# Thirty-two unused bytes per partition in front of the identity matrix, in an attention kernel with two dense layers

## The chip, the cores and the metric

The kernel runs on one core of one Trainium2 chip. The metric is the device time of one execution in microseconds (us); lower is better.

## What is computed

The reference is windowed attention followed by two dense layers, all in 32-bit floating point:

```python
scores = q @ k.T / sqrt(64)             # q, k, v: (4, 8, 768, 64): batch, heads, positions, width
scores += bias                          # a slope for each head times the distance
scores = where(is_global | is_local, scores, -1e9)   # the first 8 keys, or the last 96
a = softmax(scores)
x = (a @ v)                             # regrouped to 3072 tokens x 512
h = x @ moe_w_in;   g = h * cos(h);     y = g @ moe_w_out       # 512 -> 2048 -> 512
h = y @ moe2_w_in;  g = relu(h) ** 2;   out = g @ moe2_w_out    # 512 -> 2048 -> 512
```

## The kernel before

Nothing is scheduled by a library: every engine has its own program, written by hand (`sync`, `gpsimd`, `tensor`, `scalar`, `vector`), and the programs meet at semaphores. The tokens are cut into 6 tiles of 512 tokens (`TILES`), and the 2048 hidden columns into 16 pieces of 128 (`FC`). One step, numbered F, is one piece of one tile: 96 steps for the first layer, 96 for the second. Two steps are one `pair`.

A step has two parts on TensorE. `up(F)` (L519 to L521) makes 128 hidden columns for 512 tokens. `down(F)` multiplies them by 128 rows of the second weight matrix (L538 to L540 in the first layer, L543 to L545 in the second). Each part issues 12 matmuls of 128 rows by 128 columns by 512: 4 blocks, and 3 products each, because every operand is split into a rounded part ("hi") and the rest ("lo"), and hi*hi, hi*lo and lo*hi are added. These operands have the type float32r. A matmul takes a *stationary* operand of 128 columns, which a weight load puts into the array, and a *moving* operand of 512 columns, which streams through it. In a row of the profile, `psum<-x_parts,w_in_hi` names the moving operand first.

- `up`: moving is `x_parts` (the tokens), stationary are `w_in_hi` and `w_in_lo`.
- `down`, first layer: moving are `g_hi` and `g_lo`, stationary are `w_out_hi` and `w_out_lo`.
- `down`, second layer: moving are `w_out_hi` and `w_out_lo`, stationary are `g_hi` and `g_lo`.

The attention runs in groups G (48 of them, two heads and two blocks of 128 queries each). The first 11 run ahead of the dense layers. The others are laid between the `up` and `down` of the first 37 pairs. Their TensorE work is plain float32: transposes against `ident` (L555, L592, L595), scores (L574, out of the array `kq`) and the product with the values (L610). VectorE makes the argument of the cosine (`angle`, L955 to L961: four instructions a step), the product (`gate`, L967 or L971) and the low part (`low_g`, L975). ScalarE copies the hidden columns out of PSUM, makes the cosine and rounds. GpSimd splits the weights (L425 to L436) and normalises the probabilities (L449). In the second layer `angle` falls away.

The arrays lie in each partition of the on-chip memory in the order in which `sb(...)` names them. In the built program every array starts at a multiple of 32 bytes. `w_in_hi` starts at byte 16,512, which is 129 times 128, and `w_in_lo` at 49,280, which is 385 times 128. Seven small arrays follow (`n_words` to `half_pi`), each of which takes 32 bytes, 224 in all. So `ident` starts at byte 82,272, which is 96 bytes past a multiple of 128. Everything after it that is used here has a size that is a multiple of 128, and so starts 96 past one as well: `raw`, `x_parts0`, `x_parts1`, `w_stage`, `w_out_raw`, `w_out_hi`, `w_out_lo`, `hs`, `turns`, `act_a`, `g_hi`, `g_lo`, `y_stage`, `bias`, `probs`, `probsT`, `kq`, `vals`, `x_raw`. A slice of 512 columns is 2,048 bytes in each partition, and a stationary operand of 128 columns 512 bytes. Within the arrays of the dense layers all slices start at multiples of 512 bytes from the array's start. Within `kq` and `probs` they don't: a row of `kq` is 2,880 bytes (22.5 times 128), a slot of `probs` 928 bytes (7.25 times 128).

Of the kernel before, what the change touches and what calls it, by code (L numbers as in the profile page):

```python
# [11 lines left out]
P = 128  # L12
# [10 lines left out]
def build(nc, q, k, v, n_global, n_local, w1_in, w1_out, w2_in, w2_out, out):  # L23
# [41 lines left out]
    with ExitStack() as ctx:  # L65
        def sb(name, shape, dt=F32, where=ctx):
            return where.enter_context(nc.sbuf_tensor(name, shape, dt))
# [10 lines left out]
        fits = sb("fits", [P, 3])  # L78
        general_flag = sb("general_flag", [P, 1], I32)
        half_pi = sb("half_pi", [P, 1])  # L80
        ident = sb("ident", [P, P])
        raw = sb("raw", [P, 3, 2, 2, 2 * D])

# [1047 lines left out]
```

## Time and profile before

| what | value |
|---|---|
| time, median of 3 runs | 1290.38 us (1289.87 to 1290.68) |
| time of the profiled execution | 1287.4 us |
| its span, first to last instruction | 1285.6 us |
| outside the span | 1.8 us |
| mean granted TensorE clock | 0.996 of full speed |
| TensorE matmul (PE) busy | 1244.2 us, 97% of the span |
| VectorE (DVE) busy | 712.4 us, 55% |
| GpSimd (POOL) busy | 622.6 us, 48% |
| ScalarE (ACT) busy | 562.8 us, 44% |

The busy time of a matmul is counted from its start to its modelled end. Neighbours overlap, so how fast TensorE really goes is read from the distance between two starts, not from the duration of one.

### The profile page before, as it was taken

The page shows a single profiled execution, that of the slowest core. Times are in us where ns is not written, and L with a number is a line of the kernel's source. Part 1 is how long each engine was busy: PE and PEld are TensorE (multiplying, and loading weights), DVE is VectorE, ACT ScalarE, POOL GpSimd, SP SyncE. Part 2 cuts the span into 40 slices and gives each one's busy share as a digit, 9 for nine tenths or more (in the row PEclk, how much of TensorE's full clock was granted, in tenths as well). Part 3 has the DMA queues.
Part 4 walks back from the last instruction along what each step waited for, and adds up shares of the span by engine and source line. Part 5 has one row for each costly group of instructions (what it writes and reads, how often), then busy time and mean ns, then how long its engine had stood idle before and what let it go on. Part 6 is the DMA issues. An engine that isn't in the chain of part 4 may idle for free.

```text
span 1285.6 us, 18074 instructions
## 1 busy us (share of the span) xinstructions
PE 1244.2 (97%) x6240; PEld 991.5 (77%) x6240; DVE 712.4 (55%) x1434; ACT 562.8 (44%) x1164; POOL 622.6 (48%) x687
## 2 busy tenths in 40 slices
PE   5689999999999999999998899999999999999998
PEld 4567777777777777777776778888888888888887
DVE  6568777777767777676789962223222323222222
ACT  4655666666666666666432322222222222222221
POOL 4767455544555544555477753333333333333332
PEclk9999999999999999999999999999999999999999
DMA  4633223323222322231142332131131131321211
GB/s 122 168 87 91 74 65 101 78 64 92 80 69 77 98 73 65 69 101 49 42 143 79 97 101 67 44 114 49 49 115 47 44 115 50 93 71 44 80 49 58
DMA packets 131748, 102.01 MB, mean 79 GB/s; under 512 B 62912, under 2 KB 97856, under 8 KB 131648
## 3 DMA queue, kind: packets, MB, share of 16 engines
q1 hardware_dynamic: 131648, 100.77, 27.7%
q8 instruction: 52, 0.85, 0.3%
q14 instruction: 48, 0.39, 0.1%
HBM read 88.15 MB, written 12.58 MB: 78 GB/s over the span
## 4 chain that ended last, share of the span: by engine, by line
PE 89%; DVE 7%; ACT 2%; POOL 1%; issue 1%; DMA 0%; SPq 0%; DVEq 0%; ACTq 0%; POOLq 0%
PE psum L519 13%; PE psum L521 13%; PE psum L520 13%; PE psum L545 7%; PE psum L543 7%; PE psum L544 7%; PE psum L538 7%; PE psum L540 6%; PE psum L539 6%; PE psum L574 3%; PE psum L610 3%; PE psum L595 2%; PE psum L555 2%; DVE act_a L959 1%; DVE act_a L967 1%
## 5 line engine op out<-in xcount | busy, mean ns | idle before, releaser
L434 POOL TENSOR_SCALAR w_out_hi<-w_out_raw 128x512 fp32r<-128x512 f32 x192 | 141.3, 736 | 605.8 <-PE psum L545 320.3
L519 PE MATMUL psum<-x_parts,w_in_hi 128*128 128x512 f32 x768 | 310.5, 404 | 0.0
L521 PE MATMUL psum<-x_parts,w_in_lo 128*128 128x512 f32 x768 | 304.0, 396 | 0.0
L520 PE MATMUL psum<-x_parts,w_in_hi 128*128 128x512 f32 x768 | 303.2, 395 | 0.0
L436 POOL TENSOR_TENSOR w_out_lo<-w_out_raw,w_out_hi 128x512 fp32r<-128x512 f32 x192 | 263.0, 1370 | 16.0
L975 DVE TENSOR_TENSOR g_lo<-act_a,g_hi 128x512 fp32r<-128x512 f32 x192 | 149.2, 780 | 184.1 <-ACT g_hi L771 180.9
L761 ACT ACTIVATE hs<-psum 128x512 f32<-128x512 f32 x96 | 57.3, 597 | 364.4 <-PE psum L521 364.4
L519 PEld LDWEIGHTS psum<-x_parts,w_in_hi 128*128 128x128 f32 x768 | 144.4, 188 | 37.0 <-issue 6.5
L521 PEld LDWEIGHTS psum<-x_parts,w_in_lo 128*128 128x128 f32 x768 | 144.2, 188 | 34.3
L520 PEld LDWEIGHTS psum<-x_parts,w_in_hi 128*128 128x128 f32 x768 | 144.6, 188 | 31.7
L538 PE MATMUL psum<-g_hi,w_out_hi 128*128 128x512 f32 x384 | 158.7, 413 | 10.0 <-DVE g_lo L975 10.0
L540 PE MATMUL psum<-g_hi,w_out_lo 128*128 128x512 f32 x384 | 151.4, 394 | 0.0
L539 PE MATMUL psum<-g_lo,w_out_hi 128*128 128x512 f32 x384 | 150.8, 393 | 0.0
L545 PE MATMUL psum<-w_out_hi,g_lo 128*128 128x512 f32 x384 | 150.1, 391 | 0.0
L543 PE MATMUL psum<-w_out_hi,g_hi 128*128 128x512 f32 x384 | 149.7, 390 | 0.0
L544 PE MATMUL psum<-w_out_lo,g_hi 128*128 128x512 f32 x384 | 149.4, 389 | 0.0
L449 POOL TENSOR_SCALAR probs<-probs,row_inv 128x232 f32<-128x232 f32 (+1 forms) x192 | 134.3, 717 | 16.5 <-DVE row_inv L928 16.5
L771 ACT CAST g_hi<-act_a 128x512 fp32r<-128x512 f32 x192 | 118.4, 617 | 48.4 <-DVE act_a L971 29.0
L971 DVE TENSOR_TENSOR act_a<-hs 128x512 f32<-128x512 f32 x96 | 65.6, 702 | 88.9 <-ACT hs L761 88.9
L967 DVE TENSOR_TENSOR act_a<-hs,act_a 128x512 f32<-128x512 f32 x96 | 77.0, 837 | 60.0 <-ACT act_a L765 60.0
L759 ACT COPY hs<-psum 128x512 f32<-128x512 f32 x96 | 55.9, 582 | 117.6 <-PE psum L521 117.6
L538 PEld LDWEIGHTS psum<-g_hi,w_out_hi 128*128 128x128 f32 x384 | 72.7, 189 | 35.8 <-issue 22.3
(74 smaller groups left out, 1641.6 us busy)
## 6 DMA issues: line engine op xcount, KB each, us to landing
w_out_raw<-in_moe_w_out_dram SPq DMA_DIRECT2D x192, 256.0 KB, 2.7
vals<-in_v_dram SPq DMA_DIRECT2D x80, 112.0 KB
w_stage<-in_moe_w_in_dram SPq DMA_DIRECT2D x32, 256.0 KB, 3.1
raw<-in_k_dram SPq DMA_DIRECT2D x96, 64.0 KB, 2.4
raw<-in_q_dram SPq DMA_DIRECT2D x96, 64.0 KB, 2.2
y_dram<-y_stage SPq DMA_DIRECT2D x24, 256.0 KB, 3.6
x_raw<-y_dram SPq DMA_DIRECT2D x6, 1024.0 KB, 5.3
out_dram<-y_stage SPq DMA_DIRECT2D x24, 256.0 KB, 3.4
```

What stands on the lines that cost most here:

```text
L434: pool.tensor_scalar(hi, row, 1.0, 1.0, ALU.mult, ALU.mult).then_inc(w_out_hi_ready, 1)
L436: pool.tensor_tensor(lo, row, hi.bitcast(F32), ALU.subtract).then_inc(w_out_ready, 1)
L519: pe.matmul(to, hi, x[:, 0, c], start=(c == 0), stop=False)
L520: pe.matmul(to, hi, x[:, 1, c], start=False, stop=False)
L521: last = pe.matmul(to, lo, x[:, 0, c], start=False, stop=(c == KC - 1))
L538: pe.matmul(to, hi, g_hi[:, F % 3], start=one, stop=False)
L539: pe.matmul(to, hi, g_lo[:, F % 3], start=False, stop=False)
L540: last = pe.matmul(to, lo, g_hi[:, F % 3], start=False, stop=end)
L543: pe.matmul(to, hi, w_out_hi[:, F % 3], start=one, stop=False)
L544: pe.matmul(to, hi, w_out_lo[:, F % 3], start=False, stop=False)
L545: last = pe.matmul(to, lo, w_out_hi[:, F % 3], start=False, stop=end)
L975: dve.tensor_tensor(g_lo[:, F % 3], act_a[:, F % 4], g_hi[:, F % 3].bitcast(F32), ALU.subtract).then_inc(g_lo_ready, 1)
```

## The change

One array of 8 floats per partition is allocated ahead of `ident`. Nothing reads or writes it.

```diff
@@ -78,6 +78,7 @@
         fits = sb("fits", [P, 3])
         general_flag = sb("general_flag", [P, 1], I32)
         half_pi = sb("half_pi", [P, 1])
+        sb("pad", [P, 8])
         ident = sb("ident", [P, P])
         raw = sb("raw", [P, 3, 2, 2, 2 * D])
```

In the built program `pad` takes bytes 82,272 to 82,303, and `ident` and every array behind it move up by 32 bytes. They start at multiples of 128 afterwards (`ident` at 82,304, which is 643 times 128). `w_in_hi` and `w_in_lo`, and the small arrays, stay where they were. The slices of `kq` and of `probs` that start off a multiple of 128 within their array stay off one, or come to lie off one: the keys of a first block (byte 416 of a row of `kq`) go from 0 to 32 past a multiple in the even rows, and from 64 to 96 in the odd ones. The instructions of all five engines are the same as before, in the same order. A line number of after is one higher than the same line's of before, from L81 on.

## Rows read from the trace of the kernel before

**Rows 1.** The page: busy time of each engine, granted clock, chain that ended last.

```profile
PE 1244.2 (97%) x6240; PEld 991.5 (77%) x6240; DVE 712.4 (55%) x1434; ACT 562.8 (44%) x1164; POOL 622.6 (48%) x687
...
PE 89%; DVE 7%; ACT 2%; POOL 1%; issue 1%; DMA 0%; SPq 0%; DVEq 0%; ACTq 0%; POOLq 0%
```

**Rows 2.** Stretches, instructions of L519 alone: us, busy (x count), clock, DMA.

```profile
85.90:639.40 553.50, 127.07 (x304) 57.12 (x304) 1.00 0.28 75
639.40:746.20 106.80, 26.95 (x68) 12.92 (x68) 0.98 0.33 98
746.20:1285.60 539.40, 149.91 (x380) 71.36 (x380) 1.00 0.23 71
```

**Rows 3.** Stretches, all: us, PE, PEld, DVE, ACT, POOL busy, clock.

```profile
87.00:612.00 525.00, 525.00 (x2945) 411.11 (x2943) 378.75 (x880) 344.11 (x714) 282.86 (x320) 1.00 0.29 78
660.00:740.00 80.00, 70.62 (x296) 55.93 (x294) 77.62 (x76) 24.43 (x41) 60.94 (x52) 0.98 0.36 109
```

**Rows 4.** Timeline of PE, second layer: start us, duration us, what.

```profile
1000.43 0.39 PE L543 MATMUL psum<-w_out_hi,g_hi 128*128 128x512 f32 x1
1000.66 0.39 PE L544 MATMUL psum<-w_out_lo,g_hi 128*128 128x512 f32 x1
...
1002.92 0.40 PE L545 MATMUL psum<-w_out_hi,g_lo 128*128 128x512 f32 x1
1003.16 0.39 PE L519 MATMUL psum<-x_parts,w_in_hi 128*128 128x512 f32 x1
...
1005.72 0.40 PE L521 MATMUL psum<-x_parts,w_in_lo 128*128 128x512 f32 x1
1005.95 0.39 PE L543 MATMUL psum<-w_out_hi,g_hi 128*128 128x512 f32 x1
```

**Rows 5.** Timeline of PE where the granted clock is 0.50.

```profile
702.28 0.63 PE L538 MATMUL psum<-g_hi,w_out_hi 128*128 128x512 f32 x1
...
704.41 0.63 PE L540 MATMUL psum<-g_hi,w_out_lo 128*128 128x512 f32 x1
```

**Rows 6.** Stretches, all engines: the granted clock there (third from the end).

```profile
701.70:705.00 3.30, 3.30 (x10) 2.55 (x9) 3.10 (x5) 0.22 (x1) 0.85 (x1) 0.50 0.00 0
```

**Rows 7.** Timeline of PE among the attention groups, first layer.

```profile
408.19 0.39 PE L539 MATMUL psum<-g_lo,w_out_hi 128*128 128x512 f32 x1
...
410.48 0.39 PE L540 MATMUL psum<-g_hi,w_out_lo 128*128 128x512 f32 x1
...
411.38 0.39 PE L520 MATMUL psum<-x_parts,w_in_hi 128*128 128x512 f32 x1
...
413.71 0.39 PE L521 MATMUL psum<-x_parts,w_in_lo 128*128 128x512 f32 x1
413.94 1.04 PE L595 MATMUL psum<-ident,probs 128*116 128x128 f32 x8
```

**Rows 8.** Groups by shape: the transposes' mean duration.

```profile
L595 PE MATMUL psum<-ident,probs 128*116 128x128 f32 x320 | 46.1, 278 | 2.5 <-POOL probs L449 1.0 <-ACT probsT L702 0.8 <-ACT probsT L701 0.8
```

**Rows 9.** Timeline of PE: the scores of two neighbouring groups.

```profile
100.39 0.89 PE L574 MATMUL psum<-kq 64*128 64x128 f32 x8
115.05 0.89 PE L574 MATMUL psum<-kq 64*128 64x128 f32 x8
```

**Rows 10.** The chain that ended last, in order of time, from 640 us.

```profile
660.16 1.16 DVE turns L955
661.34 0.73 DVE turns L957
662.10 1.67 DVE act_a L959
663.79 0.99 DVE act_a L961
...
738.77 1.69 DVE g_lo L975
```

## The prediction, made before the changed kernel was run

> **What bounds the kernel now.** The page comes first. TensorE is busy for 97% of the span, and the chain of work that ended last lies on it for 89% [rows 1]. A change that adds and moves no instruction can only act through how long instructions take, so the question is how far TensorE's matmuls are from their own pace. Durations don't say that, since neighbours overlap; the starts in the timeline do.
>
> Second layer, warm clock [rows 4]: `down` starts at 1000.43 and the next `up` at 1003.16, so its 12 matmuls take 2.73 us, 227.5 ns each. `up` runs from 1003.16 to 1005.95, 2.79 us, 232.5 ns each. A step is 5.52 us. Inside `down` the gap is steadier: 1000.66 to 1002.92 is 10 gaps of 226 ns. Among the attention groups the same holds [rows 7]: 10 gaps of `down` in 2.29 us (229 ns), 10 gaps of `up` in 2.33 us (233 ns).
>
> What would be the floor? At half clock [rows 6] five gaps take 2.13 us, 426 ns each [rows 5]. That is 512 columns at 1.2 GHz (426.7 ns) and nothing more. At 2.4 GHz 512 columns are 213.3 ns. Eight transposes of 128 columns end 1.04 us after the first starts, and one lasts 278 ns, so their gap is (1040 - 278)/7 = 109 ns [rows 7, 8]: by the same count 106.7 ns, which is 256 clocks, and 2.2 ns more. So I take 213.3 + 2.5 = 215.8 ns as the pace of an undisturbed matmul of 512 columns. `down` is 12 ns above it, `up` 17 ns. **The excess is there at full clock and gone at half clock.** It is a matter of how fast the moving operand arrives, not of a fixed cost for each instruction.
>
> Where is TensorE the bound? L519 is issued four times a step, so its counts are counts of steps [rows 2]: 76 steps from 85.9 to 639.4, 17 from 639.4 to 746.2, 95 (their `up`) after that. In the first stage and the last TensorE does not stop: 525 of 525 us are busy from 87 to 612, VectorE 379 of them [rows 3]. In the middle, once the attention is over, VectorE is busy for 77.6 of 80 us against TensorE's 70.6 [rows 3], and the chain lies on VectorE from 660 to 740 us [rows 10]. A step takes 106.8/17 = 6.28 us there, not 5.5. Faster matmuls bring nothing in these 17 steps.
>
> **The change, part by part.** The `pad` itself costs nothing: no instruction touches it. What changes is the starts of operands. In `down` both operands start 96 bytes past a multiple of 128 now; in `up` the moving one does, and the stationary one (`w_in_hi`, `w_in_lo`) lies on a multiple. After the change all of them lie on multiples.
>
> The number that speaks for an effect: 2,048 bytes from a start that is 96 past a multiple touch 17 pieces of 128 bytes, from a multiple 16. 213.3 x 17/16 = 226.7 ns, and `down`'s steady gap is 226 [rows 4]. If the array's reads come in such pieces, and their rate is just what the full clock consumes, an additional piece is paid in full at 2.4 GHz and hidden at 1.2 GHz, as the half-clock gaps show [rows 5]. The sum under this reading, with 215.8 ns for all 24 matmuls of a step:
> - a step falls from 5.52 to 24 x 0.2158 = 5.18 us, by 0.34 us;
> - steps that gain: 76 + 95 = 171, and the last stage also runs four `down`s whose `up` was counted earlier. I take 173: 173 x 0.34 = 59 us;
> - the 17 steps in the middle gain 0. They could even stretch: when TensorE is quicker, VectorE's limit shows from the first of them. At their present 6.28 us nothing is added.
>
> That makes the profiled execution 1287.4 - 59 = 1228 us. The median of the runs is 3.0 us above it, so 1231 us; I say **1230**.
>
> Bounds of this term. The best is 213.3 ns flat: 24 x 0.2133 = 5.12, a gain of 0.40, times 173 = 69 us, 1221. If the pieces are of 64 bytes (33 against 32), they explain only 6.7 ns of `down`'s excess and 6.7 stay for something else: 220 ns, 5.28 us a step, 0.24 x 173 = 42 us, 1249. Nothing in the trace tells 64 from 128, since a start 96 past is off both. I take the 128, since 17/16 meets the row without a remainder.
>
> The other operations. The plain float32 matmuls take 109 ns for 128 columns [rows 7, 8], half the rate in columns of the split ones, so a late piece has time to be hidden. The scores show it: two neighbouring groups read their keys from 0 and from 64 bytes past a multiple (even and odd row of `kq`), and both take 0.89 us [rows 9]. I cost the new starts of L555, L574, L592, L595 and L610 at nothing. Their bound, gain or loss, is one piece of 13 ns for each of 8 scores, and as much for the transposes and for the values: 0.3 us a pair, 11 us in 37 pairs. I take nothing, by the equal pair. VectorE, ScalarE, GpSimd and the transfers also see every start move by 32 bytes; outside the middle stage they have 28% of slack or more [rows 3]. In the middle stage VectorE's rate is the bound, and a 1% change of it is 1 us either way.
>
> A rule that speaks against the change: by the Trainium skill (SBUF — State Buffer, the note on cachelines) the memory has lines of 16 bytes, and what costs is crossing to a new line without enough hits in the old one. A start 96 past a multiple of 128 and one on it are both starts of such a line, so by that page the change does nothing, and the time would stay at 1290.4. The 17/16 [rows 4] speaks against it, the equal pair [rows 9] for it.
>
> The same skill (TensorE: Matmul & The Clock Gate, Back-to-back issue gap) gives N/2.4 + 2.5 ns for a warm matmul, 215.8 ns for 512 columns. The trace stands 12 and 17 ns above that [rows 4]; the page would make the gain 59 us if alignment is the whole reason, and it doesn't name alignment as one.
>
> **The rivals.**
> 1. *The excess has nothing to do with the starts:* it is the price of 4-byte operands at full clock, or of reading the stationary operand beside the moving one. For it: `up`, whose stationary operand lies right already, is the slower one. Time 1290.4.
> 2. *Only the distance between the two operands counts.* The weight load of the next matmul reads beside the moving stream. In `down` both have the same remainder (96 and 96) and take 227.5 ns, in `up` 0 and 96 and take 232.5. After the change all are equal (0 and 0), and `up` falls to `down`'s pace: 12 x 5 ns = 0.06 us a step, 173 x 0.06 = 10 us, 1280.
> 3. *A stationary operand on a multiple of 128 is what costs*, slower than before. The only matmuls whose stationary operand lies on one today are the slower ones [rows 4, 7]. The change then puts `w_out` and `g` there too, and `down` goes to 232.5: again 0.06 us a step, this time lost: 1301. It decides from the first step in which TensorE is the bound, and in the middle stage it is hidden behind VectorE. Against it: no reason why an even start should be worse.
> 4. *The change doesn't do what it says.* Some slices of `kq` and `probs` don't lie on multiples of 128 afterwards. By the equal pair [rows 9] that is worth nothing, so this is no case of its own.
>
> **How the numbers follow.** The excess is gone, whole or by half (1221 to 1249): 0.40, of which 0.30 for the 128-byte reading. Rival 2: 0.13. Rival 1: 0.24. Rival 3: 0.16. Mechanisms that I don't see: 0.03 faster, 0.04 slower. A measurement of this kernel can tell about 0.2%, 2.6 us, from no change. Faster: 0.40 + 0.13 + 0.03 = 0.56; same 0.24; slower 0.20. The likeliest case has 1230 us and a range of its own of 1221 to 1249. To hold 8 in 10 the range must take in rival 2 and rival 1 as well: 1220 to 1292. Rival 3 is left out.
>
> **What would show it.** In the profile of the changed kernel, the timeline of the second layer: 12 starts of `down` and 12 of `up` in 2.59 us each would confirm the sum; 2.64 us the 64-byte reading; 2.73 both, rival 2; 2.73 and 2.79 unchanged, rival 1; 2.79 both, rival 3. The half-clock gap must stay at 426 ns, the eight transposes of a burst at 1.04 us, the scores at 0.89 us. The middle stage must stay near 6.3 us a step, or start earlier with VectorE as its bound. The prediction is wrong if the gaps don't move, or if they fall and the time doesn't, because VectorE's stage spreads over more than 17 steps.

## The result, and the profile after

| | before | after |
|---|---|---|
| median of the runs compared | 1290.23 us (4 runs, 1289.87 to 1290.68) | 1279.40 us (4 runs, 1278.30 to 1279.87) |
| profiled execution | 1287.4 us | 1279.84 us |
| its span | 1285.6 us | 1278.0 us |
| granted TensorE clock | 0.996 | 0.990 |

The ratio is 0.9915 with a 95% interval of 0.9897 to 0.9932. The change makes the kernel faster by 10.8 us, not by the 60 us of the forecast. That is the size of the second rival (1280 us).

The profiles differ by 7.6 us, the medians by 10.8. The profiled execution of before was one of its fastest: over all runs of this study before took 1287.39 to 1291.37 us. Its granted clock was 0.996; in 13 of the 15 other executions of before whose clock is on record it was 0.989 to 0.993, with spans of 1287.2 to 1289.6 us. So the profile of before holds less half clock than most of its runs. The account below is made between the two profiles, and has to be read with this in mind.

The timeline of TensorE in the second layer of the changed kernel (start us, duration us, what) answers to [rows 4]:

```profile
997.10 0.39 PE L544 MATMUL psum<-w_out_hi,g_hi 128*128 128x512 f32 x1
...
999.82 0.39 PE L520 MATMUL psum<-x_parts,w_in_hi 128*128 128x512 f32 x1
...
1002.54 0.39 PE L544 MATMUL psum<-w_out_hi,g_hi 128*128 128x512 f32 x1
```

`down` takes 2.72 us and `up` takes 2.72 us, 226.7 ns for each of the 24 matmuls. `up` was at 2.79 us, `down` at 2.73 [rows 4]. The step went from 5.52 to 5.44 us.

Stretches of L520 alone in the changed kernel (us, PE and PEld busy with counts, clock, DMA) answer to [rows 2]. The borders are the starts of the same three `down`s in both kernels, F 0, 76 and 96:

```profile
0.00:87.10 87.10, 6.54 (x16) 3.01 (x16) 0.93 0.51 133
87.10:637.80 550.70, 126.45 (x304) 57.06 (x304) 1.00 0.27 76
637.80:763.20 125.40, 31.71 (x80) 15.30 (x80) 0.96 0.30 92
763.20:1278.00 514.80, 143.15 (x368) 69.05 (x368) 1.00 0.23 72
```

And L519 alone in the kernel before, with the third border at the start of the second layer, where [rows 2] had it three steps earlier:

```profile
0.00:85.90 85.90, 6.59 (x16) 3.01 (x16) 0.97 0.52 135
...
639.40:762.80 123.40, 31.68 (x80) 15.18 (x80) 0.99 0.31 94
762.80:1285.60 522.80, 145.18 (x368) 69.10 (x368) 1.00 0.23 71
```

| stage | before | after | difference |
|---|---|---|---|
| start, to the first `down` | 85.9 us | 87.1 us | +1.2 |
| attention laid between the steps, 76 steps | 553.5 | 550.7 | -2.8 |
| the rest of the first layer, 20 steps | 123.4 | 125.4 | +2.0 |
| second layer | 522.8 | 514.8 | -8.0 |

The gain lies in the two stages in which TensorE is the bound (busy for 550.7 of 550.7 us and for 511.5 of 514.8). In the other two the profile of the changed kernel is longer, and its clock is lower: 0.93 in place of 0.97 in the start, 0.96 in place of 0.99 in the stage in which VectorE is the bound. In the latter TensorE waits for `g_lo` until 738.45, and when it goes on it is at half clock:

```profile
738.45 0.77 PE L539 MATMUL psum<-g_hi,w_out_hi 128*128 128x512 f32 x1 [3.32 <-DVE g_lo L976]
...
739.44 0.63 PE L541 MATMUL psum<-g_hi,w_out_lo 128*128 128x512 f32 x1
739.87 0.63 PE L539 MATMUL psum<-g_hi,w_out_hi 128*128 128x512 f32 x1
```

The gap there is 430 ns. The kernel before waited at the same place for 3.13 us and went on at full clock, its next start 0.30 us later:

```profile
740.59 0.47 PE L538 MATMUL psum<-g_hi,w_out_hi 128*128 128x512 f32 x1 [3.13 <-DVE g_lo L975]
740.89 0.40 PE L539 MATMUL psum<-g_lo,w_out_hi 128*128 128x512 f32 x1
```

Over 737.6 to 744.2 us the granted clock is 0.50 in the changed kernel and 1.00 in the one before. Twelve matmuls at 427 ns in place of 227 are 2.4 us, about the 2.0 us lost in this stage. The length of the wait alone doesn't tell when this happens. At another place of the same stage the kernel before waited just as long, and it was at half clock from 701.85 on:

```profile
700.54 0.47 PE L538 MATMUL psum<-g_hi,w_out_hi 128*128 128x512 f32 x1 [3.12 <-DVE g_lo L975]
...
701.85 0.63 PE L540 MATMUL psum<-g_hi,w_out_lo 128*128 128x512 f32 x1
```

Whether these two microseconds belong to the change is taken up at the end of the experiments.

### The profile page after: what moved, and what is told of

It is laid out like the page before. It is cut to its first block, busy times and chain, and to the rows that moved or that the text cites. A ratio compares the mean times of both kernels' runs of the same rounds, so it can differ in the third digit from the quotient of the medians.

```text
span 1278.0 us, 18074 instructions
## 1 busy us (share of the span) xinstructions
PE 1235.2 (97%) x6240; PEld 993.8 (78%) x6240; DVE 711.4 (56%) x1434; ACT 563.4 (44%) x1164; POOL 619.7 (48%) x687
## 4 chain that ended last, share of the span: by engine, by line
PE 88%; DVE 7%; ACT 2%; issue 1%; POOL 1%; DMA 0%; SPq 0%; DVEq 0%; ACTq 0%; POOLq 0%
PE psum L520 13%; PE psum L521 13%; PE psum L522 13%; PE psum L545 7%; PE psum L546 7%; PE psum L544 7%; PE psum L539 7%; PE psum L541 6%; PE psum L540 6%; PE psum L575 3%; PE psum L611 3%; PE psum L596 2%; PE psum L556 2%; DVE act_a L968 1%; DVE act_a L960 1%
## 5 line engine op out<-in xcount | busy, mean ns | idle before, releaser
L520 PE MATMUL psum<-x_parts,w_in_hi 128*128 128x512 f32 x768 | 307.9, 401 | 0.0
L522 PE MATMUL psum<-x_parts,w_in_lo 128*128 128x512 f32 x768 | 299.5, 390 | 0.0
L976 DVE TENSOR_TENSOR g_lo<-act_a,g_hi 128x512 fp32r<-128x512 f32 x192 | 145.0, 757 | 182.7 <-ACT g_hi L772 179.5
L520 PEld LDWEIGHTS psum<-x_parts,w_in_hi 128*128 128x128 f32 x768 | 144.4, 188 | 34.9 <-issue 6.8
L539 PE MATMUL psum<-g_hi,w_out_hi 128*128 128x512 f32 x384 | 160.1, 417 | 10.8 <-DVE g_lo L976 10.8
L968 DVE TENSOR_TENSOR act_a<-hs,act_a 128x512 f32<-128x512 f32 x96 | 81.7, 888 | 59.0 <-ACT act_a L766 58.9
```

The lines of the kernel that those rows point to most:

```text
L520: pe.matmul(to, hi, x[:, 0, c], start=(c == 0), stop=False)
L522: last = pe.matmul(to, lo, x[:, 0, c], start=False, stop=(c == KC - 1))
L539: pe.matmul(to, hi, g_hi[:, F % 3], start=one, stop=False)
L976: dve.tensor_tensor(g_lo[:, F % 3], act_a[:, F % 4], g_hi[:, F % 3].bitcast(F32), ALU.subtract).then_inc(g_lo_ready, 1)
```

## The experiments

In what follows the *distance* of a matmul is the start of its stationary operand minus the start of its moving one, in bytes, modulo 128. In the kernel before, `up` has 0 - 96, so 32, and `down` has 0. After the change both have 0.

### Both operands off a multiple of 128, by the same amount

```diff
--- after
+++ all96
+        sb("lead", [P, 24])
         w_in_hi = sb("w_in_hi", [P, KC, FF], F32R)
```

> The change, with 96 more unused bytes in front of w_in_hi: all arrays start 96 past a multiple of 128, the stationary and the moving operand of every matmul of the dense layers alike. Theory 1 (only the difference of the two remainders counts): as the changed kernel, 24 gaps of 226.7 ns in a step of the second layer, 5.44 us, and a time of 1279 us within 0.3%. Theory 2 (operands have to lie on multiples of 128): gaps of 230 ns and more, a step of 5.52 us or longer, 1290 us or more.

Measured: 1279.27 us (4 runs, 1277.63 to 1279.66), ratio to before 0.9913 (0.9897 to 0.9930), beside 0.9915 for the change. The timeline of its second layer:

```profile
1002.10 0.39 PE L545 MATMUL psum<-w_out_hi,g_hi 128*128 128x512 f32 x1
...
1004.82 0.39 PE L521 MATMUL psum<-x_parts,w_in_hi 128*128 128x512 f32 x1
...
1005.50 0.39 PE L521 MATMUL psum<-x_parts,w_in_hi 128*128 128x512 f32 x1
```

`down` takes 2.72 us, three gaps of `up` take 0.68 us: 226.7 ns, the gaps of the changed kernel. **No array that a matmul reads lies on a multiple of 128 here, and nothing is lost.** This kernel differs from the one before only in the remainder of `w_in_hi`, `w_in_lo` and the seven small arrays behind them; every other array has kept its 96. So the multiple is not the cause. The whole gain is that of `up`, whose two operands now have the same remainder, and the new starts of the attention's arrays count for nothing that shows.

It also ends the reading on which the forecast rested: a moving operand that starts 96 past a multiple touches 17 pieces of 128 bytes, as before, and takes no longer than one that touches 16.

### Other distances

Unused bytes between arrays, or a slice that starts some columns into a longer array, gave other distances:

```diff
--- after
+++ sweep32
-            x_parts = [sb(f"x_parts{i}", [P, 2, KC, NT], F32R, lay) for i in range(2)]
+            x_parts = []
+            for i, gap in enumerate((16, 24)):
+                sb(f"gap{i}", [P, gap], F32, lay)
+                x_parts.append(sb(f"x_parts{i}", [P, 2, KC, NT], F32R, lay))
...
+            sb("gap2", [P, 8], F32, lay)
             g_hi = sb("g_hi", [P, 3, NT], F32R, lay)
```

> The change, with unused bytes between the arrays, so that the start of the stationary operand minus that of the moving one is, modulo 128: 64 in the up of the even tiles (x_parts0 64 past), 96 in the up of the odd tiles (x_parts1 32 past), 32 in the down of the second layer (w_out 32 past, g 64 past), 96 in the down of the first. Theory 1 with a period of 64: gaps of 226.7 ns in the even tiles' up, 233.3 in the odd tiles' up and in the second layer's down. Theory 1 with a period of 128: the even tiles' up differs from 226.7 as well. Rival (a moving operand off a multiple costs one piece whatever the other does): all parts of the second layer slower than 226.7 ns.

```diff
--- after
+++ fine
-            x_parts = [sb(f"x_parts{i}", [P, 2, KC, NT], F32R, lay) for i in range(2)]
+            x_parts = []
+            for i, at in enumerate((4, 1)):
+                whole = sb(f"x_parts{i}", [P, 2 * KC * NT + 32], F32R, lay)
+                x_parts.append(whole[:, at:at + 2 * KC * NT].rearrange("p (a c n) -> p a c n", a=2, c=KC))
...
-            g_hi = sb("g_hi", [P, 3, NT], F32R, lay)
-            g_lo = sb("g_lo", [P, 3, NT], F32R, lay)
+            g_hi, g_lo = (sb(name, [P, 3 * NT + 32], F32R, lay)[:, 2:2 + 3 * NT].rearrange("p (a n) -> p a n", a=3)
+                          for name in ("g_hi", "g_lo"))
```

> The change, with slices that start inside a piece of 32 bytes: x_parts0 16 bytes past a multiple of 128, x_parts1 4 bytes past, g_hi and g_lo 8 bytes past; w_in and w_out lie on multiples. If the memory is read in pieces of 16 bytes, the even tiles' up stays at 226.7 ns and the odd tiles' up and the down become slower; with pieces of 32 or 64 bytes all three become slower, towards 233 ns; if starts inside a piece cost nothing, all stay at 226.7 ns.

A third kernel, fine2, is the same edit with other numbers: `x_parts` 28 and 12 columns in, `g_hi` and `g_lo` 12.

> The change, with other remainders: the stationary operand's start minus the moving one's, modulo 128, is 16 in the up of even tiles, 80 in that of odd tiles, 48 in the down of the second layer. If 0 is the best distance, all three are slower than 226.7 ns (by what the first sweep showed, 16 and 80 at 229 to 240, 48 at 230 to 235). If there is a distance at which the two reads don't meet at all, one of them falls below 226.7, towards 216.

In the timeline of sweep32 two steps of the second layer stand for the rest, one of an even tile and one of an odd:

```profile
801.98 0.39 PE L524 MATMUL psum<-x_parts,w_in_hi 128*128 128x512 f32 x1
...
804.73 0.39 PE L548 MATMUL psum<-w_out_hi,g_hi 128*128 128x512 f32 x1
```

```profile
899.87 0.40 PE L548 MATMUL psum<-w_out_hi,g_hi 128*128 128x512 f32 x1
...
902.67 0.40 PE L524 MATMUL psum<-x_parts,w_in_hi 128*128 128x512 f32 x1
...
905.48 0.40 PE L548 MATMUL psum<-w_out_hi,g_hi 128*128 128x512 f32 x1
```

Twelve gaps of `up` take 2.75 us in the even tile (distance 64) and 2.81 in the odd one (96), those of `down` 2.80 (32). The same reading in fine, an odd tile, whose moving operand starts 4 bytes past a multiple:

```profile
901.12 0.40 PE L523 MATMUL psum<-x_parts,w_in_hi 128*128 128x512 f32 x1
...
903.99 0.40 PE L547 MATMUL psum<-w_out_hi,g_hi 128*128 128x512 f32 x1
```

and in fine2, an even tile, at a distance of 16:

```profile
801.02 0.39 PE L523 MATMUL psum<-x_parts,w_in_hi 128*128 128x512 f32 x1
...
803.74 0.39 PE L547 MATMUL psum<-w_out_hi,g_hi 128*128 128x512 f32 x1
```

| distance | where (remainders: stationary, moving) | mean gap, ns |
|---|---|---|
| 0 | after, up and down (0, 0); all96 (96, 96) | 226.7 |
| 8 | fine, down (8, 0) | 232.5 |
| 16 | fine2, up of even tiles (0, 112) | 226.7 |
| 32 | before, up (0, 96); sweep32, down (64, 32) | 232.5; 233.3 |
| 48 | fine2, down (48, 0) | 231 |
| 64 | sweep32, up of even tiles (0, 64) | 229 to 230 |
| 80 | fine2, up of odd tiles (0, 48) | 231 to 233 |
| 96 | sweep32, up of odd tiles (0, 32) | 234 |
| 112 | fine, up of even tiles (0, 16) | 231.7 |
| 124 | fine, up of odd tiles (0, 4) | 239 |

The times agree: one execution each of sweep32 1296.23 us, fine 1302.54 and fine2 1289.78, beside medians of before of 1290.06, 1290.06 and 1290.18.

What follows. The expectation "a period of 64" falls, since 64 is not as good as 0. The rival of that run (a moving operand off a multiple costs a piece whatever the other does) falls by fine2: a moving operand at 112 goes at 226.7 ns. Distance 32 gives the same 233 ns with two different pairs of remainders, and distance 0 the same 226.7; the other distances were tried with one pair each. The branch of fine2 by which 0 alone is the best falls too: 16 is as good. And no distance of the ten lies below 226.7. A start 4 bytes past a multiple, which no array has by itself, is the worst, 12 ns a matmul. In fine all three parts are slower, but that doesn't make the pieces 32 or 64 bytes long, as its expectation had it: the moving operand at 112 in fine2 starts on no multiple of 32 and loses nothing.

That the distance counts modulo 128, and not modulo something longer, has only this for it: in fine2 `g_hi` and `g_lo` start 49 times 128 bytes apart, so their distances differ modulo 256, and the gaps of `down` behind either are 231 to 232 ns.

### What is left above 215.8 ns

```diff
--- after
+++ still
+                    x0, x1 = x[:, 0, c], x[:, 1, c]
+                    if i in (6, 7, 10, 11):
+                        x0, x1 = (x[:, n, c, 0:1].to_broadcast((P, NT)) for n in range(2))
+                    if i >= 8:
+                        hi, lo = (w[:, c, P * f:P * f + 1].to_broadcast((P, P)) for w in (w_in_hi, w_in_lo))
-                    pe.matmul(to, hi, x[:, 0, c], start=(c == 0), stop=False)
+                    pe.matmul(to, hi, x0, start=(c == 0), stop=False)
...
```

> The change, with operands of up in the second layer that read one address again and again (a step of 0 elements), so that its output is not the reference's: the moving one in tiles 6 and 7, the stationary one in tiles 8 and 9, both in tiles 10 and 11. down is as in the changed kernel. If the 11 ns that are left above 215.8 ns come from the two reads meeting in the memory, up falls to about 216 ns where one of the reads stays in place, or where both do. If they are a fixed price of such a matmul, up stays at 226.7 ns in all three.

The moving operand stays in place (tile 6):

```profile
802.40 0.38 PE L525 MATMUL psum<-x_parts,w_in_hi 128*128 128x512 f32 x1
...
804.99 0.39 PE L549 MATMUL psum<-w_out_hi,g_hi 128*128 128x512 f32 x1
```

2.59 us for 12, 215.8 ns: the floor that the prediction took from the transposes. With both in place the gap is 216 ns too. With the stationary one alone (tiles 8 and 9) it is 231 ns, slower than with a proper stationary operand. So the excess goes when the moving operand stays on one address, and it is not a fixed price of such a matmul. A stationary operand that stays on one address does not lower it. The time was 1274.96 us, in one execution.

`down` was not touched in this kernel, and its distance is 0. Yet behind the quicker `up` of tile 6 it takes 2.76 us (804.99 to 807.75), 230 ns a matmul: its gaps begin at 233 ns and reach 226.7 only in the last three.

```profile
807.75 0.38 PE L525 MATMUL psum<-x_parts,w_in_hi 128*128 128x512 f32 x1
```

**So the distance does not settle a gap alone; the pace of the matmuls just before counts as well.** A mean over 12 gaps that follow a part of another pace, in the table above and in the two kernels below, holds such gaps.

```diff
--- after
+++ sizes
+                    m = P if i < TILES else (64 if i < 9 else 32)
-                    pe.matmul(to, hi, x[:, 0, c], start=(c == 0), stop=False)
+                    pe.matmul(to[0:m], hi[:, 0:m], x[:, 0, c], start=(c == 0), stop=False)
...
+                        n = 384 if i < 9 else 448
-                        pe.matmul(to, hi, w_out_hi[:, F % 3], start=one, stop=False)
+                        pe.matmul(to[:, 0:n], hi, w_out_hi[:, F % 3, 0:n], start=one, stop=False)
...
```

> The change, with less work in the second layer, whose output is then not the reference's: up loads 64 stationary columns in tiles 6 to 8 and 32 in tiles 9 to 11 in place of 128 (the other hidden rows are left out), and down streams 384 columns in tiles 6 to 8 and 448 in tiles 9 to 11 in place of 512 (the rest is left out). Theory A (the weight load reads beside the moving stream and takes time from it, 13.3 ns for 128 columns): up falls to 220 ns with 64 columns and 216.7 with 32, and down is 160 + 13.3 = 173.3 ns at 384 columns and 186.7 + 13.3 = 200 at 448. Theory B (the moving stream itself arrives at 16/17 of the full rate): up stays at 226.7 ns, down takes 170.0 and 198.3 ns.

Measured: 1241.83 us in one execution. `up` takes 230 ns a matmul with 64 stationary columns and 232 with 32, where theory A has 220 and 216.7. Theory A, as it stood, falls. What fewer columns of weights do by themselves is not shown, since in every one of these tiles `down` has another pace too. `down` takes 175 ns at 384 columns, which settles at 172 to 174 in the last six of a block, and 204 at 448: above what theory B gives (170 and 198). Theory B falls too. The excess over the columns' own time (160.0 and 186.7 ns) is 13 to 15 ns at 384 and 17 to 18 at 448, beside 13.3 at 512.

```diff
--- after
+++ pace
+                    def cols(v):
+                        if i == 6:
+                            return v[:, 0:256, None].to_broadcast((P, 256, 2))
+                        if i == 7:
+                            return v[:, None, 0:256].to_broadcast((P, 2, 256))
+                        if i == 8:
+                            return v[:, None, 0:128].to_broadcast((P, 4, 128))
+                        if i == 9:
+                            return v[:, None, 0:NT:2].to_broadcast((P, 2, 256))
+                        if i == 10:
+                            return v[:, 0:256]
...
```

> The change, with another moving operand in the up of the second layer, whose output is then not the reference's. Tile 6: 256 columns, each streamed twice (half the bytes for each clock). Tile 7: 256 columns, streamed through twice. Tile 8: 128 columns, four times. Tile 9: every second column, 256, twice (the full rate over twice the bytes). Tile 10: 256 columns only. Tile 11: 128 columns only. If what is left above 215.8 ns is a matter of the rate at which new pieces are read, tile 6 falls to 216 ns, tiles 7 and 8 stay at about 227 and tile 9 is slower by far. If it is paid once where a stream starts, tiles 7 and 8 stay at 227 as well, and 256 columns take 106.7 + 13.3 = 120 ns; if it grows with the columns, 256 columns take 113 ns. Tile 11 shows what a weight load of 128 columns allows: about 109 ns.

Tile 6 (half the bytes for each clock), tile 9 (twice the bytes) and tile 10 (256 columns):

```profile
801.89 0.38 PE L535 MATMUL psum<-x_parts,w_in_hi 128*128 128x512 f32 x1
...
804.48 0.40 PE L559 MATMUL psum<-w_out_hi,g_hi 128*128 128x512 f32 x1
```

```profile
1101.19 0.63 PE L536 MATMUL psum<-x_parts,w_in_hi 128*128 128x512 f32 x1
...
1105.72 0.63 PE L537 MATMUL psum<-x_parts,w_in_lo 128*128 128x512 f32 x1
```

```profile
1171.42 0.28 PE L535 MATMUL psum<-x_parts,w_in_hi 128*128 128x256 f32 x1
...
1172.38 0.28 PE L537 MATMUL psum<-x_parts,w_in_lo 128*128 128x256 f32 x1
```

Tile 6 is at 215.8 ns (2.59 us for 12): at half the rate of bytes the excess is gone at full clock too. Tile 9 takes 453 ns (10 gaps in 4.53 us), twice 226.7. Tiles 7 and 8 stay at 226.7, so what counts is not how many different bytes are read. Tile 10 takes 120 ns (8 gaps in 0.96 us), which is 106.7 + 13.3. **The excess does not grow in step with the columns: about 13.3 ns are paid for 256 of them as for 512** (and 13 to 18 for 384 and 448, above). That twice the bytes take twice the time, and half the bytes lose the excess, fits a moving operand that is read at just the rate that the full clock consumes. With 128 columns (tile 11) the gap is 112 ns, close to the 109 ns of the transposes. The time was 1279.69 us, in one execution.

What stays open is the mechanism of these 13.3 ns and of the 6 to 12 ns that a bad distance adds. That the place of the stationary operand counts is shown: the same moving operand, at the same start, goes at 232.5 or 226.7 ns depending on where the stationary one lies (before against all96). That two reads meet in the memory is the likely reason, and is not shown: one address for all stationary columns doesn't lower the price, and a matmul without its weight load wasn't tried.

### Copies moved off VectorE, and the half clock of the middle stage

```diff
--- after
+++ actcopy
-                for c in (0, 2):
+                for c in (range(KC) if i in (4, 5) else (0, 2)):
...
-                    act.copy(y_stage[:, c], psum[:, c]).then_inc(out_copied[0], 1)
+                    act.copy(y_stage[:, c], psum[:, c]).then_inc(out_copied[c % 2], 1)
...
-                for c in (1, 3):
+                for c in (() if i in (4, 5) else (1, 3)):
```

> The change, and the two copies of each finished tile that VectorE makes out of PSUM are made by ScalarE after tiles 4 and 5. They lie in the stage in which VectorE is the bound. Theory (TensorE's waits of over 3 us there are followed by stretches at half clock, one of which the change added): four copies of 0.7 to 1.3 us leave VectorE, TensorE's waits in the stage get shorter by 2 to 3 us in all, and the half-clock stretch of 6.8 us after 737 us goes or shortens, 1.7 to 3.4 us more: 1274 to 1277 us. Rival (the waits just move to another place of VectorE's queue): 1279 us within 0.3%, with the half-clock stretches as they were.

Measured: 1277.09 us (4 runs, 1276.61 to 1277.89), ratio to before 0.9901 (0.9884 to 0.9917). Its interval overlaps that of the change (0.9897 to 0.9932), so that it beats the changed kernel is likely, not shown; it beats the kernel before. A stretch of actcopy that takes in the stage (it begins 1.4 us before the `down` of step 76, so its length can't be set beside the 125.4 us above):

```profile
636.00:760.60 124.60, 115.24 (x487) 93.87 (x486) 112.14 (x117) 40.52 (x70) 86.03 (x72) 0.96 0.31 94
```

TensorE's waits for `g_lo` fell from 10.8 us (five) to 9.4 (four), but the longest is 3.5 us, and the clock of the stage is 0.96 as in the changed kernel. The half-clock stretches only moved: 6.8 us after 696.0 and 3.4 us after 736.9, where the changed kernel has 3.4 after 699.9 and 6.8 after 737.5. The part of the theory that the half-clock time would go with them failed.

What the half clock costs, and whether the change brings it, can be read from pace. Up to the `up` of step 96 its instructions and arrays are those of the changed kernel. From the start of step 80 to the start of step 96, in before, after, pace and actcopy (us, PE, PEld, DVE, ACT, POOL busy with counts, clock, DMA):

```profile
642.10:743.40 101.30, 91.33 (x385) 72.88 (x384) 95.89 (x98) 31.30 (x53) 74.27 (x62) 0.98 0.34 102
640.50:743.70 103.20, 92.40 (x385) 74.58 (x384) 97.99 (x102) 32.09 (x54) 74.28 (x62) 0.95 0.33 100
640.90:741.90 101.00, 91.06 (x386) 73.64 (x385) 95.95 (x99) 31.40 (x53) 72.81 (x61) 0.97 0.34 102
640.10:741.60 101.50, 92.14 (x386) 74.72 (x384) 96.39 (x97) 32.44 (x55) 75.27 (x62) 0.95 0.34 102
```

Pace has one stretch at half clock there, 6.8 us from 724.3, where after has 3.4 us and 6.2. It takes 101.0 us against 103.2, and before, with 3.4 us of half clock, takes 101.3. **So the two microseconds come and go with the half clock, in the same program; the change does not have to pay them.** All96 has the same two stretches as after and takes 103.1 us. Whether the change makes them more frequent is not shown: the clock was 0.990 to 0.992 in the eight executions of after and all96, and 0.989 to 0.993 in most of those of before. Actcopy has as much half clock as after and is 1.7 us quicker over these steps, so that gain is most likely the copies'.

## Why the prediction was wrong, point by point

**Where TensorE is the bound: right.** The gain is there in the attention stage and in the second layer, and none in the 20 steps between them. In the attention stage it is 2.8 us in 76 steps, 0.04 a step, against 0.08 in the second layer. After each burst of attention work the matmuls take a few gaps to settle, as `down` does in still. Ten gaps of `up` behind four transposes, changed kernel:

```profile
411.09 0.39 PE L521 MATMUL psum<-x_parts,w_in_hi 128*128 128x512 f32 x1
...
413.38 0.40 PE L522 MATMUL psum<-x_parts,w_in_lo 128*128 128x512 f32 x1
```

2.29 us, 229 ns each; it was 2.33 us [rows 7].

**The floor of 215.8 ns: right as a floor, wrong as a goal.** Two kernels reach it (still, pace), both by not reading the moving operand at the full rate. No start of the operands came below 226.7 ns. (The transposes gave 2.2 ns above the columns' own time, and the prediction added 2.5; the difference is 1 us in its sum, and no more.)

**The reading of the excess: this step failed.** I took `down`'s 226 ns for 17 pieces in place of 16, because 213.3 x 17/16 is 226.7. In all96 there are still 17 pieces, in after 16, and both have 226.7 ns. So the term of the sum, 0.34 us a step for 24 matmuls that all fall to 215.8 ns, was 0.08 us: `up` fell by 6 ns a matmul, and the settled gap of `down` did not move. The number was a coincidence: 13.3 ns once a matmul is 1/16 of 213.3 at 512 columns only. The 256 columns of pace, at 120 ns and not 113, tell the two apart. That the excess has to do with the moving operand's rate, and goes at half clock, was right; that the start of that operand decides it was wrong. The trace of before held the warning. `up` and `down` have moving operands with the same remainder, so a count of the moving operand's pieces gives one pace for both, and [rows 4] show two. A reading that explains one of two rows and leaves the other to "something else" should not have had the largest chance. The second rival used the one thing in which `up` and `down` differ, and it was right in what matters, the two remainders being alike.

**The size of the second rival.** It gave 12 x 5 ns, 0.06 us a step, and 10 us. The step fell by 0.08: 0.07 in `up`, and 0.01 in the first and last gap of `down`, which were 231 and 235 ns and are 227. Eight us in the second layer and 2.8 in the attention stage are 10.8. Between the two profiles 3.2 us were lost again in the start and in VectorE's stage, with more half clock in both. The medians differ by 10.8 us. That this is so near the rival's 10 is in part luck: its steps gained more than it said in the second layer and less in the attention stage, and it had no term for the half clock.

**The other operations at nothing: right.** The change moves the attention's arrays and all96 leaves their remainders as they were; the two times are 0.1 us apart. The burst of eight transposes takes 1.03 us (1.04 before [rows 7]).

**The middle stage.** I added nothing there. Between the profiles it lost 2.0 us, of a kind that the prediction didn't name: 6.8 us more at half clock, which pace, the same program up to step 96, has only in part, and then it loses nothing. A step of this stage stayed near 6.3 us as the prediction asked (125.4/20 = 6.27, before 6.17). The forecast's doubt ("could even stretch") was about VectorE's share, and that did not change: VectorE is busy for 110.1 us of the 125.4, before it was 111.9 of 123.4.

**Rival 3** (a stationary operand on a multiple costs) falls with the first row of after: all are on one, and all go at the quicker pace. **Rival 1** falls with the result.

The rule of the Trainium skill's page SBUF — State Buffer (lines of 16 bytes, its note on cachelines) would have let the change do nothing. The trace disagrees: a shift by 32 bytes, two whole lines, changes `up` by 6 ns a matmul. Distance 16, one line, is as good as 0, and 124, no whole number of lines, is the worst; but 8 is no slower than 32, so the runs don't bear the lines out as the cause. The gap of 215.8 ns that the Trainium skill gives (TensorE: Matmul & The Clock Gate, Back-to-back issue gap) is met where the moving operand is not read at the full rate, and missed by 11 ns where it is.

## What to carry to other kernels

When TensorE streams 4-byte operands at full clock without pause, look at the distance between the starts of its two operands, not at whether each lies on a round number; here an equal remainder modulo 128 was worth 0.8% of the time, and an unused array of 32 bytes was enough. Read the gap between two starts and compare it between lines that differ in one thing, before a formula is fitted to one of them. Before a loss in another stage is put down to a change, compare the granted clock of the two profiles there, and look for a run of the same program in which the clock fell at other places: here 2 us of apparent loss went with the half clock, not with the change.

## What the runs showed of the hardware that was not expected

- The gap between matmuls of 512 float32r columns depends on where the stationary operand starts against the moving one: 226.7 ns at distances 0 and 16, 232.5 at 8, 229 to 234 at 32 to 112, 239 at 124. At distances 0 and 32 two pairs of starts gave the same.
- Each such matmul pays 13 to 18 ns above its columns, whatever their number: 120 ns for 256 columns, 175 for 384, 204 for 448, 226.7 for 512. It pays about 2.5 ns when the moving operand needs half the bytes for each clock, and when it stays on one address (215.8 and 216 ns).
- Every second column of a moving operand costs twice the time: 453 ns for 512 columns.
- A gap also depends on the pace before it: `down` at distance 0 takes 230 ns a matmul behind an `up` at 215.8, and needs nine gaps to come back to 226.7.
- The same instructions took 101.0 us with 6.8 us of them at half clock (pace) and 103.2 with 9.6 (after).
